# An output projection by seven half-width block products for each two chunks, its weight sums streamed from DRAM

## The reference

```python
gate = sigmoid(x @ w_gate); val = x @ w_val      # 256 -> 1536
x = (gate * val) @ w_out                          # 1536 -> 256
h = x @ w_in                                      # 256 -> 2048
out = (h - tanh(h)) @ w2_out                      # 2048 -> 256
```

## Time and profile before

| | us |
|---|---|
| median of 3 runs (2316.35 to 2319.81) | 2317.45 |
| the profiled execution | 2317.3 |
| its span | 2315.2 |
| TensorE busy | 2300.1 |
| VectorE busy | 1122.7 |
| ScalarE busy | 908.7 |
| GpSimd busy | 97.9 |

### The profile page before, as it was taken

The page is one execution under the profiler, slowest core; times in us unless marked ns, Lnnn a source line. Parts: engine busy times, 40 slices in busy tenths (PEclk is TensorE's granted clock), DMA queues, the critical chain, the costliest instruction groups (busy, mean ns, idle before and its releaser), DMA issues.

```text
span 2315.2 us, 27938 instructions
## 1 busy us (share of the span) xinstructions
PE 2300.1 (99%) x10332; PEld 1928.5 (83%) x10332; DVE 1122.7 (48%) x1639; ACT 908.7 (39%) x1548; POOL 97.9 (4%) x76
## 2 busy tenths in 40 slices
PE   8999999999999999999999999999999999999999
PEld 7888888888888888888898888888888888888888
DVE  6754545445445454454454544544544445445444
ACT  5543434334334343343343443433434434334343
POOL 3440000000000000000120000000000000000000
PEclk9999999999999999999999999999999999999999
DMA  9720010000100100001111000010010010100000
GB/s 331 220 58 10 10 18 9 9 9 9 18 9 9 18 9 9 9 7 19 37 37 17 9 9 15 3 18 9 9 18 9 9 17 1 18 9 7 10 10 8
DMA packets 211658, 61.94 MB, mean 27 GB/s; under 512 B 200224, under 2 KB 200480, under 8 KB 211616
## 3 DMA queue, kind: packets, MB, share of 16 engines
q1 hardware_dynamic: 207504, 49.21, 9.6%
q0 software_dynamic: 3312, 12.06, 1.6%
q10 hardware_dynamic: 800, 0.10, 0.0%
HBM read 49.02 MB, written 12.32 MB: 26 GB/s over the span
## 4 chain that ended last, share of the span: by engine, by line
PE 96%; DMA 1%; DVE 1%; ACT 1%; issue 0%; SPq 0%; ACTq 0%; DVEq 0%
PE up L791 55%; PE acc L791 23%; PE x_acc L791 17%; DMA qk_in<-in_k 1%; PE x_acc L817 1%; DVE sq_sum L580 1%; ACT up L434 0%; SPq L338 0%; DVE up L682 0%; DVE expd L595 0%; DVE gate_w_lo L653 0%; DVE norm L608 0%; DVE norm L616 0%; DVE g_lo L689 0%; ACT func_out L479 0%
## 5 line engine op out<-in xcount | busy, mean ns | idle before, releaser
L682 DVE TENSOR_TENSOR up<-up,func_out 128x512 f32<-128x512 f32 (+1 forms) x672 | 462.2, 688 | 655.4 <-ACT func_out L479 650.6
L479 ACT ACTIVATE func_out<-up 128x512 f32<-128x512 f32 (+1 forms) x672 | 395.6, 589 | 847.2 <-PE up L791 847.2
L689 DVE TENSOR_TENSOR g_lo<-up,g_hi 128x512 fp32r<-128x512 f32 (+1 forms) x672 | 455.7, 678 | 372.4 <-ACT g_hi L487 369.5
L487 ACT ACTIVATE g_hi<-up 128x512 fp32r<-128x512 f32 (+1 forms) x672 | 395.3, 588 | 435.2 <-DVE up L682 434.6
L791 PE MATMUL up<-x_lo,in_w_hi 128*128 128x512 f32 (+1 forms) x768 | 295.4, 385 | 0.7 <-DVE x_lo L674 0.7
L791 PE MATMUL acc<-g_lo,out_w_hi 128*128 128x512 f32 (+1 forms) x768 | 295.4, 385 | 0.5 <-DVE g_lo L689 0.5
L791 PE MATMUL up<-x_hi,in_w_hi 128*128 128x512 f32 (+1 forms) x768 | 295.4, 385 | 0.0
L791 PE MATMUL up<-x_hi,in_w_lo 128*128 128x512 f32 (+1 forms) x768 | 295.3, 385 | 0.0
L791 PE MATMUL acc<-g_hi,out_w_hi 128*128 128x512 f32 (+1 forms) x768 | 295.3, 384 | 0.0
L791 PE MATMUL acc<-g_hi,out_w_lo 128*128 128x512 f32 (+1 forms) x768 | 295.3, 384 | 0.0
L791 PE MATMUL x_acc<-g_lo,out_w_hi 128*128 128x512 f32 (+1 forms) x576 | 221.6, 385 | 0.2 <-DVE g_lo L689 0.2
(11 more groups left out here) (122 smaller groups left out, 2109.3 us busy)
## 6 DMA issues: line engine op xcount, KB each, us to landing
v_in<-in_v SPq DMA_DIRECT2D x176, 64.0 KB, 2.2
out_rows<-out_sb SPq DMA_DIRECT2D x176, 64.0 KB, 1.8
qk_in<-in_q SPq DMA_DIRECT2D x29, 384.0 KB, 4.0
qk_in<-in_k SPq DMA_DIRECT2D x29, 384.0 KB, 5.9
w_stage<-in_moe_w_out POOLq DMA_DIRECT2D x4, 512.0 KB, 4.2
w_stage<-in_moe_w_gate POOLq DMA_DIRECT2D x3, 512.0 KB, 7.5
out_sb<-in_moe_w_val POOLq DMA_DIRECT2D x3, 512.0 KB, 7.6
out_sb<-in_moe_w_out POOLq DMA_DIRECT2D x3, 512.0 KB, 4.5
```

What stands on the lines that cost most here:

```text
L479: act.activation(func_out[:, half, cut], src[:, cut], func).then_inc(func_made, 1)
L487: act.activation(hi[:, i % SLOTS, cut], product_bank(kind, i)[:, cut], ACT.Copy).then_inc(g_hi_made, 1)
L682: dve.tensor_tensor(bank_cut, bank_cut, func_out[:, half, cut], ALU.mult if kind == "U" else ALU.subtract).then_inc(prod_made, 1)
L689: dve.tensor_tensor(lo[:, i % SLOTS, cut], product_bank(kind, i)[:, cut], hi[:, i % SLOTS, cut].bitcast(F32), ALU.subtract).then_inc(g_lo_ ...
```

## The change

The output projection of the second network takes its chunks in pairs. The two chunks of hidden values (256 rows) and the tile's columns form a 2 x 2 of blocks: G11 and G12 the even chunk's left and right half of the tile, G21 and G22 the odd chunk's. The weights form A11, A12, A21, A22. In place of eight block products it forms seven, of sums of blocks (a scheme of Strassen's kind, after Winograd): S1 to S4 of weights, T1 to T4 of hidden values. Each product is half a tile wide (256 columns, or 192 in the short tiles) and is still made by `product3`. The seven products of all eight pairs of a tile are summed in seven half banks: `acc` and `x2_acc`. At the end of the tile ScalarE copies the first to SBUF, and VectorE makes the four output blocks of them by seven additions (`sum_out`) before it transposes.

- TensorE: per pair 21 matmuls of half width in place of 12 of full width. The order is U(j), D(j-3) (LEAD is 3), D(9), D(10), D(11), U12, P0, P1, U13, then P(2m), P(2m+1), O(m-1), then U14, O(7). The banks of `up` and their waits are given anew.
- VectorE: per pair the even chunk's product is made as two halves (the right one goes to SBUF, `kept`), the odd one whole; four sums T1 to T4 and two remainders follow. All of these have one operand in PSUM.
- ScalarE: per pair two tanh, `hi` of G11 and of G21 with G22, and two copies that make `hi` of T1, T2 and of T3, T4.
- GpSimd: `lo` of the T sums, two instructions of 512 elements per pair. For w2_out its four pieces are no longer split, but combined (`combine_piece`): each makes the S sums and the pairs of two chunk pairs in `g2` and `t_sums`, and stores them to a DRAM tensor `w2_sums`. The first waits for the second attention matrix, since `g2` and `t_sums` lie where the early buffers lay.
- SP: loads each pair's 14 blocks (7168 bytes a partition, 917,504 bytes) from `w2_sums` into a ring of two slots, for every tile anew.
- ScalarE and SP wait in tile 0 for all four stores of GpSimd.
- In SWITCH the first five folds of the second batch stand in one block before P0, the sixth after P1.

```diff
@@ -53,8 +53,12 @@
     T_END = N - (TILES_BATCH - 1) * T
     Q = 32
     TB = T // Q
-    LEAD = 2
+    LEAD = 3
     SLOTS = 3
+    PAIRS = J2 // 2
+    PAIR_SLOTS = 2
+    PRODUCTS = 7
+    PAIR_SUMS = 7
     assert B == 2 and T_END % Q == 0 and TILES_BATCH > 3
     assert J1 % SLOTS == 0
 
...
@@ -88,41 +89,61 @@
         return t * T - b * (T - T_END)
 
     def body_chunks(tile):
-        ahead = [("U", J1 + n) for n in range(AHEAD[tile])]
-        final = [("U", J1 + AHEAD[tile] + n) for n in range(AFTER[tile])]
-        return ([("U", j) for j in range(LEAD, J1)] + ahead + [("P", i) for i in range(J2)] + final)
+        usual = [("U", j) for j in range(LEAD, J1)]
+        second = [("P", i) for i in range(J2)]
+        if tile in LONG:
+            return (usual + [("U", J1)] + second[:2] + [("U", J1 + 1)] + second[2:]
+                    + [("U", J1 + 2)])
+        return usual + second + ([("U", J1 + n) for n in range(LEAD)] if tile == SWITCH else [])
 
...
+            def load_w2(t, m):
+                sp.dma_start(w2_ring[:, m % PAIR_SLOTS, :].bitcast(F32), w2_sums[m]
+                             ).then_inc(ring_loaded[m % PAIR_SLOTS], 16)
+
+            def load_first_w2(t, first=False):
+                if first:
+                    sp.wait_ge(att_made, B * KC)
+                    for slot in range(PAIR_SLOTS):
+                        sp.wait_ge(comb_stored[slot], 16 * (COMBS // PAIR_SLOTS))
+                for m in range(PAIR_SLOTS):
+                    if not first:
+                        sp.wait_ge(down_made, nth_pair(t - 1, PAIRS - PAIR_SLOTS + m))
+                    load_w2(t, m)
+
+            def load_rest_of_w2(t):
+                for m in range(PAIR_SLOTS, PAIRS):
+                    sp.wait_ge(down_made, nth_pair(t, m - PAIR_SLOTS))
+                    load_w2(t, m)
...
+            def combine_piece(n):
+                q = n - WHOLE
+                pool.wait_ge(w_loaded[n % 2], 16 * (n // 2 + 1))
+                if q >= PAIR_SLOTS:
+                    pool.wait_ge(comb_stored[q % PAIR_SLOTS], 16 * (q // PAIR_SLOTS))
+                elif q == 0:
+                    pool.wait_ge(att_made, B * KC)
+                rows = w_stage[n % 2].rearrange("p (r a f) -> p r a f", r=2, a=2)
...
+                done = 13 * q
+                pool.tensor_tensor(whole[:, :, S1 - S1], a21, a22, ALU.add).then_inc(comb_step, 1)
+                pool.tensor_tensor(whole[:, :, S3 - S1], a11, a21, ALU.subtract).then_inc(comb_step, 1)
+                for o, a in ((A11, a11), (A12, a12), (A22, a22)):
+                    pool.tensor_scalar(hi[:, :, o], a, 1.0, 0.0, ALU.mult, ALU.add
+                                       ).then_inc(comb_step, 1)
+                pool.wait_ge(comb_step, done + 1)
+                pool.tensor_tensor(whole[:, :, S2 - S1], whole[:, :, S1 - S1], a11, ALU.subtract
+                                   ).then_inc(comb_step, 1)
+                for o, a in ((A11, a11), (A12, a12), (A22, a22)):
+                    pool.wait_ge(comb_step, done + 3 + o)
+                    pool.tensor_tensor(lo[:, :, o], a, hi[:, :, o].bitcast(F32), ALU.subtract
+                                       ).then_inc(comb_step, 1)
...
+                pool.wait_ge(w_split, n + 1)
+                pool.dma_start(w2_sums[2 * q:2 * q + 2].rearrange("r p f -> p r f"),
+                               g2[:, q % PAIR_SLOTS, :].rearrange("p (r f) -> p r f", r=2
+                                                                  ).bitcast(F32)
+                               ).then_inc(comb_stored[q % PAIR_SLOTS], 16)
+                load_next(n)
+
+            def split_t_sums(t, tile=USUAL):
+                half = width(tile) // 2
+                for m in range(PAIRS):
+                    hi, lo = pair_part(m, HI), pair_part(m, LO)
+                    for first in (T1, T3):
+                        cut = slice(first, first + 2)
+                        pool.wait_ge(t_hi_made, 2 * PAIRS * t + 2 * m + (first - T1) // 2 + 1)
+                        pool.tensor_tensor(lo[:, cut, 0:half], t_sums[:, first - T1:first - T1 + 2, 0:half],
+                                           hi[:, cut, 0:half].bitcast(F32), ALU.subtract
+                                           ).then_inc(t_lo_made, 1)
...
+            with pool.Fori(0, TILES_BATCH - 1) as t:
+                split_t_sums(t)
...
+            def hi_of_pair(t, m, tile, first=False):
+                half = width(tile) // 2
+                hi = pair_part(m, HI)
+                if m >= PAIR_SLOTS:
+                    act.wait_ge(down_made, nth_pair(t, m - PAIR_SLOTS))
+                elif not first:
+                    act.wait_ge(down_made, nth_pair(t - 1, PAIRS - PAIR_SLOTS + m))
+                act.wait_ge(prod_made, nth(t, ("P", 2 * m), tile))
+                act.activation(hi[:, G11, 0:half], product_bank("P", 2 * m, tile)[:, 0:half], ACT.Copy
+                               ).then_inc(g_hi_made, 1)
+                act.wait_ge(prod_made, nth(t, ("P", 2 * m + 1), tile))
+                act.activation(hi[:, G21:G22 + 1, 0:half],
+                               product_bank("P", 2 * m + 1, tile)[:, 0:2 * half]
+                               .rearrange("p (o c) -> p o c", o=2), ACT.Copy
+                               ).then_inc(g_hi_made, 1)
+
...
+                if first:
+                    for slot in range(PAIR_SLOTS):
+                        act.wait_ge(comb_stored[slot], 16 * (COMBS // PAIR_SLOTS))
+                for m in range(PAIRS):
+                    func_of(t, "P", 2 * m, tile)
+                    if m > 1:
+                        hi_of_t_sums(t, m - 1, T3, tile)
+                    func_of(t, "P", 2 * m + 1, tile)
+                    hi_of_pair(t, m, tile, first)
+                    hi_of_t_sums(t, m, T1, tile)
+                    if m == 0:
+                        if tile in LONG:
+                            func_of(t, "U", J1 + 1, tile)
+                        hi_of_t_sums(t, m, T3, tile)
...
+            def products_of_pair(t, m, tile, first_pair=False):
+
+                half = width(tile) // 2
+                even, odd = ("P", 2 * m), ("P", 2 * m + 1)
+                bank, func = product_bank(*even, tile), func_half(t, *even, tile)
+                dve.wait_ge(func_made, nth(t, even, tile))
+                if not first_pair:
+                    dve.wait_ge(t_sums_made, 4 * (PAIRS * t + m))
+                dve.tensor_tensor(bank[:, 0:half], bank[:, 0:half], func[:, 0:half], ALU.subtract)
+                dve.tensor_tensor(kept[:, 0:half], bank[:, half:2 * half], func[:, half:2 * half],
+                                  ALU.subtract).then_inc(prod_made, 1)
+                bank, func = product_bank(*odd, tile), func_half(t, *odd, tile)
+                dve.wait_ge(func_made, nth(t, odd, tile))
+                dve.tensor_tensor(bank[:, 0:2 * half], bank[:, 0:2 * half], func[:, 0:2 * half],
+                                  ALU.subtract).then_inc(prod_made, 1)
...
+                done = 4 * (PAIRS * t + m)
+                dve.wait_ge(g_hi_made, n_even)
+                if not first_pair:
+                    dve.wait_ge(t_lo_made, 2 * (PAIRS * t + m))
+                dve.tensor_tensor(t1, g12, g11, ALU.subtract
+                                  ).then_inc(t_sums_made, 1)
+                dve.tensor_tensor(lo[:, G11, 0:half], g11, hi[:, G11, 0:half].bitcast(F32),
+                                  ALU.subtract).then_inc(g_lo_made, 1)
+                dve.wait_ge(g_hi_made, n_odd)
+                dve.wait_ge(t_sums_made, done + 1)
+                dve.tensor_tensor(t2, g22, t1, ALU.subtract
+                                  ).then_inc(t_sums_made, 1)
+                dve.tensor_tensor(t3, g22, g12, ALU.subtract
+                                  ).then_inc(t_sums_made, 1)
+                dve.wait_ge(t_sums_made, done + 2)
+                dve.tensor_tensor(t4, t2, g21, ALU.subtract
+                                  ).then_inc(t_sums_made, 1)
+                dve.tensor_tensor(lo[:, G21:G22 + 1, 0:half],
+                                  odd[:, 0:2 * half].rearrange("p (o c) -> p o c", o=2),
+                                  hi[:, G21:G22 + 1, 0:half].bitcast(F32), ALU.subtract
+                                  ).then_inc(g_lo_made, 1)
+
...
+                dve.wait_ge(down_made, nth_pair(t, PAIRS - 1))
+                dve.tensor_tensor(u2, m6, first_sum[:, cut], ALU.add).then_inc(out_summed, 1)
+                dve.tensor_tensor(m1, m2, first_sum[:, cut], ALU.add).then_inc(out_summed, 1)
+                dve.wait_ge(out_summed, done + 1)
+                dve.tensor_tensor(u3, m7, u2, ALU.add).then_inc(out_summed, 1)
+                dve.tensor_tensor(u4, m5, u2, ALU.add).then_inc(out_summed, 1)
+                dve.wait_ge(out_summed, done + 3)
+                dve.tensor_tensor(spare, m5, u3, ALU.add).then_inc(out_summed, 1)
+                dve.wait_ge(out_summed, done + 4)
```

(54 more changed lines are left out.)

486 lines of the change are left out of this document (302 added, 184 removed).

## The result

| | before | after |
|---|---|---|
| median, us | 2316.9 (2314.22 to 2319.81, 4 runs) | 2344.03 (2343.12 to 2344.66, 4 runs) |
| ratio | | 1.0117 [1.0099, 1.0134] |
| the profiled execution, its span | 2317.3, 2315.2 | 2343.1, 2341.3 |
| mean granted clock | 0.999 | 0.991 |

The change makes the kernel 1.2% slower. The forecast was 2340 with a range of 2308 to 2364.

A forecast was written before the change was run, and what follows sets the result against it. TensorE, busy 99% of the span, was taken as the bound. Terms -35.2 + 3.7 + 8.6 + 0.7 + 39.0 + 1.7 + 4.4 gave +22.9 us, so 2340 us; own range 2326 to 2354, full range 2308 to 2364.

The forecast's parts named there:

- the stall: First tile: TensorE waits before P2 for GpSimd's combined w2_out sums and their last store, gated by the second attention matrix; +39.0 us.
- the clock: Tile 0, after TensorE's long pause: matmuls run at the 1.2 GHz level for a while, +1.7 us.
- The narrow products: Output projection, long tiles: 21 matmuls of 256 columns at 120 ns replace 12 of 512 per pair, -35.2 us.
- the load floor: Narrow matmuls: weight load allows nothing under 110 ns, taken for 192 columns; as rival at 256 columns, 2303 us, chance 0.13.
- U13: Next tile's second chunk waits for U12's banks with only P0 and P1 between: 0.39 us in 22 tiles, +8.6 us.
- GpSimd's thin cover: Pair stage: GpSimd's last remainder is ready 0.3 to 0.45 us before TensorE's O(m-1) needs it, so hidden.
- the rival: Pair stage: GpSimd's remainder comes late each pair, 2358 to 2417 us; sign, a usual tile near 94 us; chance 0.08.
- The ring: SP's loads of each pair's weight sums from DRAM take 5.3 us, needed 7.96 us later: hidden, no cost.
- The end: After the last P: GpSimd's chain, seven dependent sums, transposes and SP's stores take 4.9 us more, +4.4 us as a term.
- The rival that the stall can be filled: First tile: sums made faster or other work fills the pause, so TensorE doesn't stall; 2300 us, chance 0.05.
- short tiles: Two 384-wide tiles: 192-column halves take 2.31 us per pair against 2.08, +3.7 us.
- the switch tile: There P3 and the next tile's U3 each come about 0.35 us late, +0.7 us.

## Why the prediction was right, point by point

- **The sign and its cause.** Right, by its own chain. The terms were the stall at +39.0 and the clock at +1.7 against -35.2 of matmul time. Removing the gate gave 26.5 us back, nearly the whole loss. No rival took part: the stall was there, the pitch was 120 ns, GpSimd was on time. That the profiled span is only 3.2 us above the forecast's is in part luck: the front of that trace was 3.1 us early, by chance as far as the traces show.
- **The stall.** Forecast: gate at 154.9, four pieces in 46.1 us, store 7.9, P2 at 211.8. Measured: 152.6, 45.4, 6.3, P2 at 207.0. TensorE's pause began at 169.4 (172.8 forecast), 3.4 us early, and the gate came 2.3 early, so 1.1 of the two doesn't cancel. Against it stand 0.7 for the combine, 1.6 for the store and 0.1 for the chain behind it. In length 37.6 against 39.0: the store's rate was underrated. 512 KB at 4.2 us and 352 GB/s gave 7.9; 1.84 MB in 6.26 is 293 GB/s with all overhead.
- **The clock.** Twelve matmuls, most of them 0.427 apart, 2.4 us lost, against 1.7. The forecast took it from the mean over the first 58 us; the pause cost 12 x (0.427 - 0.227). The Trainium skill ("TensorE: Matmul & The Clock Gate", Back-to-back issue gap) gives N / 1.2 for this level, 0.427 at 512 columns: the trace agrees.
- **The narrow products.** The pitch of 0.120 is exact at 256 columns, 0.1105 at 192 (the load floor, as taken). By the Trainium skill's N/2.4 + 2.5 of the same section, which the page gives for a single matmul on its own, they would take 0.109 and 0.0825; the trace shows neither. What the sum lacked is the step from narrow to wide: 2.75 in place of 2.72 us for the twelve wide ones of each pair, with 2.51 in place of 2.52 for the narrow. A pair saves 0.18 us, not 0.20: 176 x 0.18 = -31.7 in place of -35.2. This is the mis-sized term with the largest effect.
- **U13.** 0.41 us a tile, forecast 0.39, but in 20 tiles and not in 22: 8.2 us. In the two tiles ahead of the short ones P2 and P3 lose 0.59 and 0.64 instead. 0.34 a tile came back where the wait was changed.
- **GpSimd's thin cover.** 0.33 us measured, 0.3 to 0.45 forecast. It held. The price of the rival held too: one more instruction a pair made a usual tile 94.47 us, where the forecast named 94 as its sign.
- **The ring.** Costed at nothing, and nothing was measured, to 0.2%.
- **The end.** From the end of the last P to the end of the span: 13.3 us, before 8.5; +4.8, forecast 4.9. What it missed stands a little earlier: the 1.3 us ahead of the first O of the last tile, where VectorE's remainder of P1 is awaited and no U13 covers it. The forecast priced U13 only where it stands and not where it is missing. The gap of 1.03 that is called "issue" too stands ahead of P0 of the last tile, where the row of the matmul itself names VectorE's remainder of x2; both kernels have it.
- **The rival that the stall can be filled.** It stood at 0.05 and 2300, with the argument that "the gate is the attention matrix itself". This step failed. I took over from the code that the gate was needed, and did not look at the addresses. Without it, in another order and with U13's wait changed the change gives 2304, 12 us faster than before. As a forecast of this kernel it did no harm; as a statement on what the change can be worth it was wrong. That rival's price of 2300 looks closer than it was: some 6 of the 12 us are U13's wait, which it did not take away.

The sum of the measured terms (-31.7, short tiles +4.1, U13 +8.2, P2 and P3 in two tiles +1.2, stall +37.6, clock +2.4, end +4.8 and +1.3, front -3.1) is +24.8 us, against 26.1 of span. 1.3 us are not assigned, the late first chunks behind the switch tile (0.34 at 1255.09, 0.11 at 1258.33) among them. Of the 0.7 forecast there, P3's half is not in the trace.

## What to carry to other kernels

A saving spread over 22 tiles (1.0 us each) was eaten by one wait in the first; when a change moves set-up work to another engine, follow that work's last result to the first instruction that needs it, and test each wait in it: here one that guards nothing cost 26.5 us. An engine that works 26% of the span can be 0.33 us from setting the pace of every step, so count its cover in the stage and not its share. Moving a long list to GpSimd beside a VectorE that another chain needs has a price of its own, in waits that look like slow instructions of VectorE.

## What was not expected of the hardware

- A VectorE instruction on 2 elements took 5.83 us beside nine GpSimd instructions without a pause between. Over the whole combine VectorE's instructions took 8.6 to 8.8 us more than their shortest in the three traces without waits between GpSimd's instructions, 3.1 to 3.5 with a wait between each and 3.6 with a few. Two of 0.68 us took 2.92 and 1.90 beside the splits of w_in. What is seen is that VectorE comes in when GpSimd stops for a wait on its own last instruction. VectorE's products and remainders of 512 elements, with an operand in PSUM, kept their 0.69 to 0.70 us beside the combine, all but one of 1.73 us right behind a held instruction. The Trainium skill ("SBUF — State Buffer", SBUF: two separate sides) describes an exclusive lock on a shared pair of ports, held for one whole instruction; the trace agrees with the lock, but here it is not given up between GpSimd's instructions.
- A wide matmul behind narrow ones is slower for a few instructions: the starts are 0.234, 0.236, 0.229, 0.232, 0.230 us apart and then 0.227, so twelve of 512 columns take 2.75 us in place of 2.72 and six 1.39 in place of 1.36, with no wait on record. Less what the narrow ones behind a wide one gain, this costs 0.02 us a pair, 3.5 us over 176 pairs.
